# FFT filter and two MLPs: the transform's second transposition by transfers through device memory, the inverse with its table stationary, tables loaded once

## The chip, the cores and the metric

The kernel runs on 1 core of a Trainium2 chip. The metric is the time of one execution on the device in microseconds (us). In text and rows PE is TensorE, PEld its weight load, DVE is VectorE, ACT ScalarE, POOL GpSimd and SP SyncE. SP computes nothing here: it issues nearly all transfers, one after the other, in the order of its program.

## The reference

```python
def reference(x, filt_r, filt_i, ...):      # x (2, 3008, 256)
    X = np.fft.rfft(x, axis=1)
    Y = X * (filt_r + 1j * filt_i)[None]
    y = np.fft.irfft(Y, n=3008, axis=1).reshape(6016, 256)
    h = y @ moe_w_in                        # 256 -> 2048
    y = np.maximum(0.01 * h, h) @ moe_w_out # 2048 -> 256
    r = np.maximum(y @ moe2_w_in, 0.0)
    return (r * r) @ moe2_w_out
```

## The kernel before

The program is written out by hand, engine by engine. Each engine runs its own list in order, and semaphores are all that ties the lists together. An instruction that waits holds back everything behind it on its engine.

**The transform** works on 3008 = 64 x 47 points, in two halves of 128 channels, with both batches side by side.
- `over_n1(c, half)` (L763) multiplies four columns of X by a 128x128 DFT table `DM[:, 0]`; ACT (half 0) and DVE (half 1) copy the results to `TT1A`/`TT1B`. There are 12 chunks `c` per half (`CH`).
- Then come 32 units `i` (`UNITS`), 16 (`PAIRS`) for each half. A unit has, on PE, `turn` (L779, four transpositions), `spectrum` (L792, two matmuls with the forward table `TB` stationary) and `inverse` (L803, four matmuls with the data `YF` stationary and the inverse table moving). ACT copies `turn`'s result (`turned`, L444) and `inverse`'s (`back`, L448, into `UT`). DVE's `filtered` (L631) multiplies the spectrum by the filter in three instructions (L642, L646, L649), and POOL adds the two products (L373). PE's loop body `i` is `turn(i+3)`, `spectrum(i+2)`, `inverse(i)`.
- `turn_back(c)` (L815) transposes four 128x128 blocks of `UT`, ACT copies them to `V` (L455), `sequence(c)` (L824) multiplies them by the last DFT table, and DVE copies the result to `YT` (L652). There are 24 such chunks. Nine of half 0 stand in the middle, at `i == TURN` (16); a few stand in the last units; those up to c = 20 follow the loop; and the last three (`fill`, L968) stand between groups of the first MLP slot (`FILL` = 21).

**The weights of MLP 1** are prepared during the transform, for k = 0 to 7. SP loads `WIF` (L216), POOL forms sums in four instructions (`wi_sums`, L281: L287, L289, L292, L293), ACT rounds (`wi_round`, L459), and POOL forms the low part in three instructions (`wi_split`, L295: 384, 256 and 256 columns). The tables `WI_LOAD`, `WI_SUM`, `WI_HI` and `WI_LO` (L155 to L159) say after which unit each stands. For k = 0 to 5 the rounding stands at least two units ahead of the first split that needs it; k = 2 and 3 are done in the middle, beside the nine chunks.

**SP** keeps five filter slots. `load_filter(i)` (L204) waits for `inverse(i-5)` and loads the unit's table (`TB`, 182 KB) and its filter (`FL`, 224 KB). The tables come in twice, once for each half.

**The MLPs** are 96 slots of PE groups (L893 to L966). The first group needs POOL's linear forms of `YT` (`x_forms`, L328), ACT's roundings and DVE's differences (`x_split0`, L674).

Of the kernel before, what the change touches and what calls it, by code (L numbers as in the profile page):

```python
# [6 lines left out]
N1, N2 = 64, 47  # L7
# [17 lines left out]
FSLOTS = 5  # L25


def fft_mlp_kernel(nc, x, filt, dft, tab, w1i, w1o, w2i, w2o, out):
# [18 lines left out]
    YF = at("YF", [KR, 3, B, 2 * 128], f32, 24 * KB)  # L47
    XF = at("XF", [KR, 2, B, 2 * 128], f32, 30 * KB)
    UT0 = at("UT0", [128, B, MH, 128], f32, o_wo)
    V = at("V", [128, 2, 512], f32, o_wo + 24 * KB)  # L50
# [6 lines left out]
    UT1 = at("UT1", [128, B, MH, 128], f32, o_g)  # L57
    o_tb = [o_s + 2 * TBW * 4 * i for i in range(4)] + [o_x + 13824]
    TB = [at(f"TB{i}", [KR, 2, TBW], f32, o_tb[i]) for i in range(FSLOTS)]
# [24 lines left out]

    wi2 = nc.dram_tensor("wi2", [128, KU, 2, 7, 128], f32).ap()
    wo2 = nc.dram_tensor("wo2", [128, KU, 2, 2 * D], f32).ap()

    with ExitStack() as ctx:
        def sem(name):
# [8 lines left out]
        ft_in = [sem(f"ft_in{g}") for g in range(FSLOTS)]  # L98
        s2_ps = sem("s2_ps")
# [7 lines left out]
        v_ps = sem("v_ps")  # L107
        v_sb = sem("v_sb")
        y_ps = sem("y_ps")
        y_sb = sem("y_sb")  # L110
# [42 lines left out]
        TURN = PAIRS  # L153

        WI_LOAD = {0: 0, 2: 1, 6: 2, 9: 3, 12: 4, 14: 5, 20: 6, 23: 7}  # L155
        WI_SUM = {3: (0, 0), 4: (0, 1), 5: (1, 0), 6: (1, 1), 18: (4, 0), 19: (4, 1), 20: (5, 0), 21: (5, 1)}
        WI_HI = {5: 0, 7: 1, 20: 4, 22: 5}
        WI_LO = {7: (0, 0), 8: (0, 1), 9: (0, 2), 10: (1, 0), 11: (1, 1), 12: (1, 2),
                 22: (4, 0), 23: (4, 1), 24: (4, 2), 25: (5, 0), 26: (5, 1), 27: (5, 2)}  # L159
        FILL = 2 * CH - 3  # L160
# [4 lines left out]
        EARLY = CH - 3  # L165
        UT = [UT0, UT1]
# [30 lines left out]
        def _(sp):  # L197
# [6 lines left out]
            def load_filter(i):  # L204
                if i >= FSLOTS:
                    sp.wait_ge(u_ps, i - FSLOTS + 1)
                sp.dma_start(TB[i % FSLOTS][:, :, :], tab[:, i % PAIRS, :, :]).then_inc(ft_in[i % FSLOTS], 16)
                sp.dma_start(FL[:, i % FSLOTS, :, :], filt[:, i, :, :]).then_inc(ft_in[i % FSLOTS], 16)

            load_x(0)  # L210
            load_x(1)
            for i in range(UNITS):
                load_filter(i)
                if i - FSLOTS in WI_LOAD:
                    k = WI_LOAD[i - FSLOTS]
                    sp.dma_start(WIF[:, k, 0:4, :], w1i[:, k, :, :]).then_inc(wi_raw[k], 16)  # L216
# [57 lines left out]
        def _(pool):  # L274
# [53 lines left out]
            def x_forms(p, part):  # L328
# [4 lines left out]
                if part == 0:  # L333
                    if p == 0:
                        pool.wait_ge(y_sb, CH + 2)
                        pool.wait_ge(s2_ps, UNITS)
                    elif p == 1:
                        pool.wait_ge(y_sb, 2 * CH)
                    else:
                        pool.wait_ge(p3_ps, (p - 1) * KU)  # L340
# [29 lines left out]
            for i in range(UNITS):  # L370
# [3 lines left out]
                if i in WI_SUM:  # L374
                    wi_sums(*WI_SUM[i])
                if i in WI_LO:
                    wi_split(*WI_LO[i])
                if i == TURN:
                    for k in (2, 3):
                        for part in range(2):  # L380
                            wi_sums(k, part)
                    for k in (2, 3):
                        for part in range(3):
                            wi_split(k, part)
# [5 lines left out]
            for k in (6, 7):  # L390
                for part in range(2):
                    wi_sums(k, part)
            x_forms(0, 0)
# [3 lines left out]
            for k in range(2):  # L397
                wo_split(k)
                for part in range(3):
                    wi_split(6 + k, part)  # L400
# [27 lines left out]
        def y_bank(c):  # L428

            return c % 2 if c < FILL else 4 + c % 2  # L430
# [6 lines left out]
        def _(act):  # L437
# [10 lines left out]
            def back(i):  # L448

                j = 2 * (i % PAIRS)  # L450
                act.wait_ge(u_ps, i + 1)
                nc.scalar.activation(UT[i // PAIRS][:, :, :, 4 * j:4 * j + 8],
                                     PS[:, 4 + i % 2, 0:4 * K2].rearrange("p (b q m) -> p b m q", b=B, m=MH), ACT.Copy).then_inc(u_sb, 1)

            def turned_back(c):  # L455
                act.wait_ge(v_ps, c + 1)
                nc.scalar.activation(V[:, c % 2, :], PS[:, 6 + c % 2, :], ACT.Copy).then_inc(v_sb, 1)
# [22 lines left out]
            def x_round0(i):  # L480

                d, t = X0[i]
                if i == 0:
                    act.wait_ge(y_sb, CH + 2)
# [21 lines left out]
            for i in range(UNITS):  # L506
                if i + 3 < UNITS:
                    turned(i + 3)
                if i == TURN:
                    turned_back(0)  # L510
                if i == UNITS - 2:
                    turned_back(EARLY)
                    turned_back(EARLY + 1)
                if i == UNITS - 1:
                    turned_back(EARLY + 2)
                back(i)
                if i in WI_HI:
                    wi_round(WI_HI[i])
                if i == TURN:
                    for c in range(1, EARLY):  # L520
                        turned_back(c)
# [586 lines left out]
```

## Time and profile before

| | |
|---|---|
| median of 3 runs | 1106.75 us (1105.6 to 1107.02) |
| the profiled execution | 1106.98 us |
| its span | 1105.2 us |
| granted clock, mean | 1.000 |
| PE busy | 99% of the span |
| DVE, ACT, POOL busy | 70%, 52%, 27% |
| transform, to the first MLP group | 127.9 us |

The span runs from the first to the last instruction; the profiled execution's own time is 1.8 us longer. PE's busy share is near full in every stretch, so a wait on PE is a wait of the whole program. The other engines' shares are means over stages of different kinds. Times in the rows below are counted from the span's start.

### The profile page before, as it was taken

The numbers are of one execution on the slowest core, as the hardware profiler recorded it, in microseconds if no ns is written. First come the engines' busy times: TensorE is split into PE (matmuls) and PEld (weight loads), VectorE is DVE, ScalarE is ACT, GpSimd is POOL, SyncE is SP. The second block draws the span as 40 slices with busy tenths as digits, with TensorE's granted clock in tenths as the row PEclk, the third lists the DMA queues.
The fourth block names the chain that finished last, engine by engine and source line by source line (L and its number), as shares of the span: only waits on it lengthen the run. The fifth ranks groups of instructions, "written<-read, shape, count | busy, mean of one in ns | idle before, by whom it ended". The sixth has DMA issues, their size and how long they took to land.

```text
span 1105.2 us, 14486 instructions
## 1 busy us (share of the span) xinstructions
PE 1094.6 (99%) x5312; PEld 929.9 (84%) x5312; DVE 776.6 (70%) x1193; ACT 569.5 (52%) x991; POOL 301.3 (27%) x291
## 2 busy tenths in 40 slices
PE   8999999999999999999999999999999999999998
PEld 8899978888888888888888888888888888888887
DVE  2979787777677676776676667667666676677665
ACT  3455655565455555555554454554554554554543
POOL 0778833224334234234121120120120210210000
PEclk9999999999999999999999999999999999999999
DMA  8545110011211211212244200000000000000000
GB/s 311 165 150 171 45 43 1 1 50 46 48 51 51 60 44 41 65 39 51 58 157 148 81 1 1 39 1 1 39 1 1 36 1 1 39 1 1 39 1 36
DMA packets 64086, 58.34 MB, mean 53 GB/s; under 512 B 40592, under 2 KB 50960, under 8 KB 64016
## 3 DMA queue, kind: packets, MB, share of 16 engines
q1 hardware_dynamic: 63872, 57.23, 16.8%
q8 instruction: 42, 0.69, 0.3%
q14 instruction: 28, 0.23, 0.1%
q10 hardware_dynamic: 144, 0.20, 0.0%
HBM read 39.71 MB, written 17.69 MB: 52 GB/s over the span
## 4 chain that ended last, share of the span: by engine, by line
PE 98%; DVE 1%; DMA 0%; POOL 0%; issue 0%; ACT 0%; DVEq 0%
PE PS L879 16%; PE PS L880 16%; PE PS L881 16%; PE PS L887 13%; PE PS L889 13%; PE PS L888 13%; PE PS L799 2%; PE PS L811 2%; PE PS L770 2%; PE PS L832 2%; PE PS L788 1%; PE PS L821 1%; DMA DM<-in_dft 0%; POOL YF L373 0%; DVE GF L718 0%
## 5 line engine op out<-in xcount | busy, mean ns | idle before, releaser
L575 ACT ACTIVATE GH<-GF 128x512 fp32r<-128x512 f32 (+1 forms) x384 | 238.7, 622 | 224.8 <-DVE GF L720 116.3
L726 DVE TENSOR_TENSOR GL<-GF,GH 128x512 fp32r<-128x512 f32 (+1 forms) x384 | 259.6, 681 | 108.1 <-ACT GH L575 101.4
L880 PE MATMUL PS<-GL,WOH 128*128 128x512 f32 (+1 forms) x768 | 296.4, 386 | 0.0
L879 PE MATMUL PS<-GH,WOH 128*128 128x512 f32 (+1 forms) x768 | 296.3, 386 | 0.0
L881 PE MATMUL PS<-GH,WOL 128*128 128x512 f32 (+1 forms) x768 | 296.1, 386 | 0.0
L887 PE MATMUL PS<-XH,WIH 128*128 128x512 f32 (+1 forms) x672 | 260.1, 387 | 1.2 <-DVE GF L711 0.8
L889 PE MATMUL PS<-XH,WIL 128*128 128x512 f32 (+1 forms) x672 | 259.2, 386 | 0.0
L694 DVE TENSOR_TENSOR GF<-PS,GF 128x512 f32<-128x512 f32 (+1 forms) x96 | 65.3, 680 | 170.5 <-ACT GF L546 170.5
L881 PEld LDWEIGHTS PS<-GH,WOL 128*128 128x128 f32 x768 | 144.1, 188 | 27.7
L880 PEld LDWEIGHTS PS<-GL,WOH 128*128 128x128 f32 x768 | 144.1, 188 | 27.6
L879 PEld LDWEIGHTS PS<-GH,WOH 128*128 128x128 f32 x768 | 144.2, 188 | 27.6
L887 PEld LDWEIGHTS PS<-XH,WIH 128*128 128x128 f32 x672 | 126.1, 188 | 27.9 <-ACT SN L553 2.1
L888 PE MATMUL PS<-YL,WIH 128*128 128x512 f32 (+1 forms) x384 | 148.0, 385 | 0.0
L889 PEld LDWEIGHTS PS<-XH,WIL 128*128 128x128 f32 x672 | 126.1, 188 | 24.2
L546 ACT ACTIVATE GF<-PS 128x512 f32<-128x512 f32 (+1 forms) x96 | 56.6, 590 | 172.5 <-PE PS L881 172.5
L718 DVE SCALAR_TENSOR_TENSOR GF<-GF 128x512 f32<-128x512 f32 (+1 forms) x192 | 137.3, 754 | 1.7
L720 DVE SCALAR_TENSOR_TENSOR GF<-GF 128x512 f32<-128x512 f32 (+1 forms) x192 | 121.7, 674 | 1.7
L888 PE MATMUL PS<-XL,WIH 128*128 128x512 f32 (+1 forms) x288 | 111.1, 386 | 0.0
L360 POOL TENSOR_TENSOR YL<-YT,XH 128x1024 fp32r<-128x1024 f32 (+1 forms) x22 | 51.7, 2352 | 137.5 <-DVE GL L726 137.5
L569 ACT ACTIVATE GF<-PS 128x512 f32<-128x512 f32 (+1 forms) x96 | 56.7, 591 | 58.4 <-PE PS L889 58.4
L888 PEld LDWEIGHTS PS<-YL,WIH 128*128 128x128 f32 x384 | 72.1, 188 | 13.5
L344 POOL TENSOR_TENSOR XT<-YT 128x512 f32<-128x512 f32 (+1 forms) x12 | 15.2, 1268 | 188.3 <-DVE GL L726 185.2
(64 smaller groups left out, 1062.4 us busy)
## 6 DMA issues: line engine op xcount, KB each, us to landing
FL<-in_filt SPq DMA_DIRECT2D x32, 224.0 KB, 3.4
TB<-in_tab SPq DMA_DIRECT2D x32, 182.0 KB, 2.9
X<-in_x SPq DMA_DIRECT2D x8, 512.0 KB, 8.9
out_y<-YT SPq DMA_DIRECT2D x4, 1024.0 KB, 4.3
wi<-PWH SPq DMA_DIRECT2D x16, 224.0 KB, 2.5
wi<-PWL SPq DMA_DIRECT2D x16, 224.0 KB, 3.1
WIH<-wi SPq DMA_DIRECT2D x8, 448.0 KB, 3.4
WIL<-wi SPq DMA_DIRECT2D x8, 448.0 KB, 4.4
```

Of the source, the lines that this page charges most:

```text
L569: nc.scalar.activation(GF[:, g_slot(n), 0:width(s)], PS[:, XB[s % 2], 0:width(s)], ACT.Copy).then_inc(h_sb[UD], 1)
L575: nc.scalar.activation(GH[:, g, 0:width(s)], GF[:, g, 0:width(s)], ACT.Copy).then_inc(g_hi[kind], 1)
L694: nc.vector.tensor_tensor(h, PS[:, YB, 0:w], h, ALU.add).then_inc(h_sb[UA], 1)
L718: nc.vector.scalar_tensor_tensor(h, h, 0.01, h, ALU.mult, ALU.max).then_inc(g_sb[kind], 1)
L720: nc.vector.scalar_tensor_tensor(h, h, 0.0, h, ALU.max, ALU.mult).then_inc(g_sb[kind], 1)
L726: nc.vector.tensor_tensor(GL[:, g, 0:w], GF[:, g, 0:w], GH[:, g, 0:w].bitcast(f32), ALU.subtract).then_inc(g_lo[kind], 1)
L879: nc.tensor.matmul(acc, wh, xh, start=first, stop=False)
L880: nc.tensor.matmul(acc, wh, xl, start=False, stop=False)
L881: return nc.tensor.matmul(acc, wl, xh, start=False, stop=last)
L887: nc.tensor.matmul(acc, wh, xh, start=first, stop=False, skip_group_check=not first)
L888: nc.tensor.matmul(acc, wh, lo, start=False, stop=False, skip_group_check=not first)
L889: return nc.tensor.matmul(acc, wl, xh, start=False, stop=True, skip_group_check=not first)
```

## The change

- `inverse` has the inverse table stationary and `YF` moving: two matmuls of 256 columns in place of four of 96. Its result lies in PSUM with the point index on 96 partitions. ACT copies 96x512 (before 128x384) into `U`, a ring of four slots (`USLOTS`).
- `turn_back`, `UT` and ACT's `turned_back` are gone. SP stores each unit's `U` to device memory (`store_u`, 196 KB) and loads it back turned (`load_v`, six transfers of 512 KB for each half, in runs of 1 KB) into `V0` and `V1`. V0's loads stand beside units 18 to 28; V1's stand behind the loop, and the first of them waits for all stores of half 1.
- All 24 `sequence` chunks follow the loop (20 ahead of the MLP, `FILL` = 20, four in its first slot). They take two PSUM banks in turn; DVE copies the even chunks and ACT the odd ones.
- The 16 tables are loaded once (`TB`, 26.6 KB per partition, over the first batch of X). The first load waits for `over_n1`.
- The weights' preparation is spread evenly: `wi_sums(k)` at i = 5k+1 and 5k+2, `wi_round(k)` at 5k+3, `wi_split(k, 0)` at 5k+4, its other parts at 5k+5 and 5k+8, for k = 0 to 5. k = 6 and 7 follow the loop. Weight load k+1 stands at i = 5k+2; that of k = 7 stands behind the loads of V1.

```diff
@@ sync
             def load_filter(i):
+                if i < PAIRS:
+                    if i in (0, PAIRS - 2):
+                        for half in range(2):
+                            sp.wait_ge(n1_ps[half], CH // 2 if i == 0 else CH // 2 + 1)
+                    sp.dma_start(TB[:, i, :, :], tab[:, i, :, :]).then_inc(tb_in[i], 16)
                 if i >= FSLOTS:
                     sp.wait_ge(u_ps, i - FSLOTS + 1)
-                sp.dma_start(TB[i % FSLOTS][:, :, :], tab[:, i % PAIRS, :, :]).then_inc(ft_in[i % FSLOTS], 16)
                 sp.dma_start(FL[:, i % FSLOTS, :, :], filt[:, i, :, :]).then_inc(ft_in[i % FSLOTS], 16)
+            def load_w1i(k):
+                sp.dma_start(WIF[:, k, 0:4, :], w1i[:, k, :, :]).then_inc(wi_raw[k], 16)
+            def store_u(i):
+                half, u = i // PAIRS, i % PAIRS
+                sp.wait_ge(u_sb, i + 1)
+                sp.dma_start(zu[half, :, 2 * u:2 * u + 2, :], U[:, i % USLOTS, :, :]).then_inc(z_out[half][i % USLOTS], 16)
+            def load_v(half, g):
+                if g == 0:
+                    for u in range(USLOTS):
+                        sp.wait_ge(z_out[half][u], 16 * (PAIRS // USLOTS))
+                by_q = zu[half].rearrange("(m q) j e -> (q j) m e", q=4)
+                sp.dma_start(V[half][:, 4 * g:4 * g + 4, :, :].rearrange("p m b d -> p m (b d)"),
+                             by_q[:, 4 * g:4 * g + 4, :]).then_inc(v_in[half][g], 16)
...
+            for i in range(FSLOTS):
+                load_filter(i)
+            load_w1i(0)
             for i in range(UNITS):
-                load_filter(i)
...
+                if i + FSLOTS < UNITS:
+                    load_filter(i + FSLOTS)
+                store_u(i)
+                if i % 5 == 2 and i // 5 + 1 < KU:
+                    load_w1i(i // 5 + 1)
+                g = (i - PAIRS - 2) // 2
+                if i % 2 == 0 and 0 <= g < MH // 4:
+                    load_v(0, g)
+            for g in range(MH // 4):
+                load_v(1, g)
+            load_w1i(KU - 1)
+            sp.wait_ge(y_ps, CH)
             for k in range(KU):
-                sp.wait_ge(v_ps, CH)
-                if k >= 4:
-                    sp.wait_ge(y_ps, 2 * CH)
                 sp.dma_start(WOF[:, k, :], w1o[:, k, :]).then_inc(wo_raw[k], 16)
@@ scalar
             def back(i):
                 act.wait_ge(u_ps, i + 1)
...
+                if i >= USLOTS:
+                    n = i - USLOTS
+                    act.wait_ge(z_out[n // PAIRS][n % USLOTS], 16 * (n % PAIRS // USLOTS + 1))
+                nc.scalar.activation(U[:, i % USLOTS, :, :].rearrange("p k e -> p (k e)"), PS[0:K2, 4 + i % 2, :], ACT.Copy).then_inc(u_sb, 1)
...
+            for c in range(1, FILL, 2):
+                y_copy(c)
+                if c == 5:
+                    wi_round(6)
+                if c == 7:
+                    wi_round(7)
@@ tensor
             def inverse(i):
...
-                for b in range(B):
-                    for k in range(2):
-                        col = (2 * b + k) * K2
-                        mm = nc.tensor.matmul(PS[:, 4 + i % 2, col:col + K2], YF[:, i % 3, b, 128 * k:128 * k + 128],
-                                              TB[i % FSLOTS][:, k, KR:], start=True, stop=True)
+                for k in range(2):
+                    mm = nc.tensor.matmul(PS[0:K2, 4 + i % 2, 256 * k:256 * k + 256].rearrange("p (b d) -> p b d", b=B),
+                                          TB[:, i % PAIRS, k, KR:], YF[:, i % 3, :, 128 * k:128 * k + 128], start=True, stop=True)
...
+            def sequence(c):
+                half, g, b = c // CH, c % CH // 2, c % 2
+                pe.wait_ge(v_in[half][g], 16)
                 if c >= 2:
-                    pe.wait_ge(v_sb, c - 1)
+                    pe.wait_ge(y_sb[c % 2], c // 2)
...
+            pe.wait_ge(s2_sb, UNITS)
+            for c in range(FILL):
                 sequence(c)
```

Three places show how the order moves; the prediction speaks of each.

SP, from the last units to the weights of the second matrix, before (`TB`, `FL` tables and filter; `WIF`, `WOF` weights of MLP 1):

```order
L207 DMA TB_63<-in_tab 112x416
L208 DMA FL<-in_filt 112x512
L216 DMA WIF<-in_w1i 128x512
L207 DMA TB_64<-in_tab 112x416
L208 DMA FL<-in_filt 112x512
...
L222 DMA WOF<-in_w1o 128x512 x8
```

and of the change:

```order
L214 DMA zu<-U 96x512
L209 DMA WIF<-in_w1i 128x512
L214 DMA zu<-U 96x512
L221 DMA V_54<-zu 128x4x256
L214 DMA zu<-U 96x512 x3
L221 DMA V_55<-zu 128x4x256 x6
L209 DMA WIF<-in_w1i 128x512
L244 DMA WOF<-in_w1o 128x512 x8
```

The last `WIF` load (k = 7) stood ahead of the last three tables and filters, whose rows the ... leaves out in part; it now stands behind the last stores and the six loads of `V1`.

ACT, behind the loop, before (`V` copies of the transposed blocks, `WIH` the roundings of k = 6 and 7, `XH` of the MLP's input):

```order
L457 ACTIVATE V<-PS 128x512 x2
L461 ACTIVATE WIH<-WIF 128x896
L457 ACTIVATE V<-PS 128x512
L461 ACTIVATE WIH<-WIF 128x896
L457 ACTIVATE V<-PS 128x512
L487 ACTIVATE XH_73<-YT 128x512
```

and of the change (`YT` copies of the odd chunks):

```order
L483 ACTIVATE U<-PS 96x512 x3
L489 ACTIVATE YT<-PS 128x512 x3
L493 ACTIVATE WIH<-WIF 128x896
L489 ACTIVATE YT<-PS 128x512
L493 ACTIVATE WIH<-WIF 128x896
L489 ACTIVATE YT<-PS 128x512
```

ACT now frees a PSUM bank of `sequence` on both sides of the rounding of k = 7 (the second `WIH` row): the three copies and the single one ahead of it are those of c = 1, 3, 5 and 7, the one behind it is that of c = 9.

POOL in the loop, before (`YF` the addition of one unit, `WIL` splits), units 6 to 8:

```order
L373 TENSOR_TENSOR YF<-YF,XF 112x512
L292 TENSOR_TENSOR WIF<-WIF 128x128
L293 TENSOR_TENSOR WIF<-WIF 128x128
L373 TENSOR_TENSOR YF<-YF,XF 112x512
L299 TENSOR_TENSOR WIL<-WIF,WIH 128x384
L373 TENSOR_TENSOR YF<-YF,XF 112x512
```

and of the change, units 7 to 10:

```order
L314 TENSOR_TENSOR WIF<-WIF 128x128
L315 TENSOR_TENSOR WIF<-WIF 128x128
L396 TENSOR_TENSOR YF<-YF,XF 112x512
L321 TENSOR_TENSOR WIL<-WIF,WIH 128x256
L396 TENSOR_TENSOR YF<-YF,XF 112x512
L321 TENSOR_TENSOR WIL<-WIF,WIH 128x384
L396 TENSOR_TENSOR YF<-YF,XF 112x512
```

The 384-column split is the first part of a pair of weights, and waits for ACT's rounding of them. It now stands behind the addition of unit 9, one unit behind the one after which ACT rounds (8); it stood behind that of unit 7, two behind (5).

## Rows read from the trace of the kernel before

**Rows 1.** The page's busy line: us, share of the span, instructions.
```profile
PE 1094.6 (99%) x5312; PEld 929.9 (84%) x5312; DVE 776.6 (70%) x1193; ACT 569.5 (52%) x991; POOL 301.3 (27%) x291
```

**Rows 2.** Busy time by stretch, then granted clock, DMA share, GB/s.
```profile
45.47:56.00 10.53, 10.53 (x79) 9.54 (x79) 10.06 (x15) 6.72 (x12) 10.06 (x12) 1.00 0.71 216
```

**Rows 3.** Chain that ended last, 60 to 130 us: start, us, what.
```profile
70.08 0.44 PE PS L821 x4
70.52 0.89 PE PS L832 x8
...
83.03 0.87 PE PS L811 x8
...
107.01 0.87 PE PS L811 x8
...
114.01 0.92 PE PS L832 x8
...
127.24 0.91 PE PS L832 x8
```

**Rows 4.** Timeline of the last units: start, us, engine, line, instruction.
```profile
102.05 0.68 DVE L649 TENSOR_TENSOR XF<-PS,FL 48x512 f32<-48x512 f32 x1
102.81 1.28 POOL L373 TENSOR_TENSOR YF<-YF,XF 112x512 f32<-112x512 f32 x1 [0.31 <-DVE XF L649]
104.47 1.08 PEld L811 LDWEIGHTS PS<-TB,YF 112*128 112x128 f32 x8
104.68 1.03 PE L811 MATMUL PS<-TB,YF 112*128 112x96 f32 x8
105.75 0.49 ACT L452 ACTIVATE UT<-PS 128x384 f32<-128x384 f32 x1 [1.14 <-PE PS L811]
105.99 1.03 PE L799 MATMUL PS<-S,TB 96*112 96x256 f32 x4
106.19 0.59 ACT L446 ACTIVATE S<-PS 96x512 f32<-96x512 f32 x1
```

**Rows 5.** Timeline, weight preparation: a split in the loop, sums, a rounding.
```profile
99.58 1.00 POOL L299 TENSOR_TENSOR WIL<-WIF,WIH 128x384 fp32r<-128x384 f32 x1
...
112.71 0.45 POOL L287 TENSOR_TENSOR WIF<-WIF 128x128 f32<-128x128 f32 x1
...
114.19 0.46 POOL L293 TENSOR_TENSOR WIF<-WIF 128x128 f32<-128x128 f32 x1
...
117.18 0.94 ACT L461 ACTIVATE WIH<-WIF 128x896 fp32r<-128x896 f32 x1
```

**Rows 6.** DMA issues: queue, kind, count, KB each, median us to landing.
```profile
FL<-in_filt SPq DMA_DIRECT2D x32, 224.0 KB, 3.4
WIF<-in_w1i SPq DMA_DIRECT2D x8, 256.0 KB, 3.8
PVF<-in_w2o SPq DMA_DIRECT2D x16, 128.0 KB, 2.1
wo<-PVH SPq DMA_DIRECT2D x16, 128.0 KB, 1.7
```

**Rows 7.** DMA, 234 to 236 us: store of PVL, load of PVF, runs of 1 KB.
```profile
DMA packets 288, 0.26 MB, mean 131 GB/s; under 512 B 32, under 2 KB 288, under 8 KB 288
q1 hardware_dynamic: 288, 0.26, 39.6%
```

**Rows 8.** DMA, 15 to 27 us in 40 slices: X, then tables and filters.
```profile
GB/s 396 437 382 423 410 423 396 410 396 437 382 423 445 324 354 254 296 292 269 338 304 299 304 304 289 361 276 272 331 302 315 268 322 299 337 223 125 48 34 0
```

**Rows 9.** Timeline of the start: copies of the first N1 chunks.
```profile
6.79 0.60 ACT L442 ACTIVATE TT1A<-PS 128x512 f32<-128x512 f32 x1 [4.33 <-PE PS L770]
8.50 0.69 DVE L629 COPY TT1B<-PS 128x512 f32<-128x512 f32 x1 [8.50 <-PE PS L770]
10.21 0.60 ACT L442 ACTIVATE TT1A<-PS 128x512 f32<-128x512 f32 x1 [2.82 <-PE PS L770]
11.30 0.69 DVE L629 COPY TT1B<-PS 128x512 f32<-128x512 f32 x1 [2.11 <-PE PS L770]
```

**Rows 10.** Timeline: one sequence chunk, its DVE copy, POOL's first linear form.
```profile
117.81 1.06 PE L832 MATMUL PS<-DM,V 128*128 128x128 f32 x8
...
118.91 0.69 DVE L658 COPY YT<-PS 128x512 f32<-128x512 f32 x1 [0.64 <-PE PS L832]
...
119.68 1.28 POOL L344 TENSOR_TENSOR XT<-YT 128x512 f32<-128x512 f32 x1 [3.13 <-DVE YT L658]
```

**Rows 11.** Timeline: a wait of PE in the second MLP slot.
```profile
140.61 0.50 PE L887 MATMUL PS<-XH,WIH 128*128 128x512 f32 x1 [0.81 <-DVE GF L711]
```

More of the change, by code:

```diff
@@ L98, in fft_mlp_kernel @@
         ft_in = [sem(f"ft_in{g}") for g in range(FSLOTS)]
+        tb_in = [sem(f"tb_in{u}") for u in range(NJ // 2)]
         s2_ps = sem("s2_ps")
@@ L373, in _ @@
                 nc.gpsimd.tensor_tensor(YF[:, i % 3, :, :], YF[:, i % 3, :, :], XF[:, i % 2, :, :], ALU.add).then_inc(yf_sb, 1)
[L374 to L384, printed above, removed]
+                k, n = i // 5, i % 5
+                if n in (1, 2) and k < WI_EARLY:
+                    wi_sums(k, n - 1)
+                if n == 3 and k >= 1:
+                    wi_split(k - 1, 2)
+                if n == 4:
+                    wi_split(k, 0)
+                if n == 0 and k >= 1:
+                    wi_split(k - 1, 1)
+            wi_split(WI_EARLY - 1, 2)
             def beside_psum(s):
                 pool.wait_ge(g_lo[UB], s)
-            for k in (6, 7):
+            for k in range(WI_EARLY, KU):
                 for part in range(2):
                     wi_sums(k, part)
+            for k in range(WI_EARLY, KU):
+                for part in range(3):
+                    wi_split(k, part)
             x_forms(0, 0)
@@ L396, in _ @@
             x_split(0, 3)
-            for k in range(2):
-                wo_split(k)
-                for part in range(3):
-                    wi_split(6 + k, part)
+            wo_split(0)
+            wo_split(1)
             for k in range(2, KU):
@@ L508, in _ @@
                     turned(i + 3)
[L509 to L515, printed above, removed]
-                back(i)
[L517 to L521, printed above, removed]
-                        if c in (4, 5):
-                            wi_round(c - 2)
-            for c in range(CH, FILL + 1):
-                turned_back(c)
-                if c in (CH + 1, CH + 2):
-                    wi_round(c - CH + 5)
-                if CH + 3 <= c < CH + 6:
-                    x_round0(c - CH - 3)
-                if c == CH + 6:
+                back(i)
+                if i % 5 == 3 and i // 5 < WI_EARLY:
+                    wi_round(i // 5)
+            for c in range(1, FILL, 2):
[4 more added lines that the diff above has]
+                    wi_round(7)
+                if c == CH + 3:
+                    x_round0(0)
+                    x_round0(1)
+                if c == CH + 5:
+                    x_round0(2)
                     x_round(0, 2)
@@ L669, in _ @@
                     filtered(i + 2)
-                if i == TURN:
-                    for c in range(EARLY):
-                        sequence(c)
             def x_split0(i):
@@ L681, in x_split0 @@
                                         ALU.subtract).then_inc(x0_lo, 1)
-            for c in range(EARLY, FILL):
-                sequence(c)
-                if CH + 5 <= c < CH + 9:
-                    x_split0(c - CH - 5)
+            for c in range(0, FILL, 2):
+                y_copy(c)
+                if c == CH + 4:
+                    x_split0(0)
+            x_split0(1)
+            x_split0(2)
+            x_split0(3)
             def whole_a(s):
@@ L957, in down @@
                     pe.wait_ge(evac[t], p)
-                elif first:
-                    pe.wait_ge(y_sb, 2 * CH)
-                    pe.wait_ge(v_sb, 2 * CH)
+                elif first and t == 1:
+                    for y in y_sb:
+                        pe.wait_ge(y, CH)
                 pe.wait_ge(g_lo[kind], s + 1)
@@ L1044, in dft_tables @@
         inv[r, 0, inp], inv[IM + r, 0, inp] = w * c, -w * s
+    inv[:] = inv.reshape(KR, NJ, 2, 2, MH).transpose(0, 1, 4, 2, 3).reshape(KR, NJ, K2)
     return dft.astype(np.float32), tab.astype(np.float32), rows
```

141 lines of the change are left out of this document (47 added, 94 removed).

## The prediction

> **What bounds the kernel now.** I read the page's busy lines first: PE is busy for 99% of the span [rows 1], so a gain must take work from PE, and any wait that PE gets is paid in full. The change ends with the transform, so next I read the chain of waits there [rows 3]. It is PE nearly throughout. A unit of the loop takes 2.17 us. A chunk of the last stage takes 0.44 us for its four transpositions and 0.89 us for its matmuls. The last inverse ends at 114.0 us (I call this moment T), and the last chunk ahead of the MLPs ends at about 127.9. The timeline of a unit [rows 4] shows how near the others are. DVE's last product of unit 27 ends at 102.73, POOL adds until 104.09, and the inverse's weight load starts at 104.47, so POOL may come 0.38 us late. ACT copies the inverse's result at 105.75. The stretches [rows 2] show DVE and POOL at 96% in the loop and the DMA engines at 0.71 with 216 GB/s, so they are full near 305 GB/s.
>
> **The sum, part by part.** All times stand against the profiled execution (1106.98 us, 0.2 above the median).
>
> 1. The inverse with its table stationary streams 2 x 256 columns. It should take what `spectrum`, of the same form, takes: 1.03 us in the timeline, as the four of 96 columns do [rows 4]. It costs and gives nothing. ACT's copy becomes 0.59 for 0.49.
>
> 2. The transpositions go: 24 x 0.44 = 10.6 us of PE. By stages: the middle block (nine chunks of 1.33) goes from the loop, 12.0, and 0.4 more in the last units. Of what stands there most was filling, since the last additions wait for DVE, so no more than that is gained. T falls from 114.0 to 101.5. Then 20 chunks stand behind T.
>
> 3. The tables' first load waits until PE has six chunks of both halves behind it, near 17 us. X itself loads until about 20 us [rows 8], the table is small, and five pairs of table and filter (2.1 MB at 300 GB/s) are there by 27 us, when the first spectrum is due. Cost: nothing. If X were not the cover, the first units would wait.
>
> 4. POOL waits for ACT's rounding. Counted from the DVE end of unit 5k+3: its inverse starts at +1.74 and its copy at +3.02 [rows 4]. The copy takes 0.5 (it overlaps the next by 0.1) and the rounding 0.94 [rows 5], so it ends near +4.5. POOL has done its addition of unit 5k+4 at +3.5 and waits a us for this. Split (1.0) [rows 5], addition (1.28) and hand-overs end at +6.8, and the inverse of unit 5k+5 wants to start at +6.08. So PE waits 0.7 us, five times (k = 0 to 4) = 3.5. For k = 5 the split falls in the last units, where nothing is left ahead of PE: 1.0. Bounds: 0, if ACT's part hides somehow, and 0.9 each time. T = 106.0.
>
> 5. The weight load of k = 7 stands behind V1's six loads, its sums wait for it, ACT's `wi_round(7)` waits for the sums, and behind that stands ACT's copy of chunk 9, which frees the bank of chunk 11. So PE runs chunks 0 to 10 until about T+10.3 and stops. From T: copy 0.6; last store 2.0 (a 128 KB store lands in 1.7 [rows 6], 64 KB more are 0.2); V1's loads are issued at T+2.75. Six of 524 kB and the weights' 262 kB are 3.41 MB. The nearest rows, transfers in runs of 1 KB, moved 0.26 MB in 39.6% of 2 us, which is 330 GB/s [rows 7]: 10.3 us. What a load takes around its transfer is 2.1 less 0.4 = 1.7 [rows 6]. The weights land at T+14.8. Ends: 8.5 us at X's 400 GB/s, 11.4 at the tables' 300 [rows 8]. I take 330, since the run length is the same. Then four sums, 1.94 from the first's start to the last's end, rounding 0.94 [rows 5], copy 0.6: chunk 11 starts at T+18.3 and PE has stood for 8 us. This eats the gain nearly alone.
>
> 6. Chunks 11 to 19. PE needs 0.89 each, but two banks in turn bind it: matmuls 1.06, then DVE's copy 0.69 [rows 10], with hand-overs 1.8 to 1.95 for two chunks. I take 0.93: 8.4 us.
>
> 7. PE's clock after the stand. The only start from rest in the trace is the first: the copies of N1 chunks follow each other at 1.71 us (6.79, 8.50, 10.21), then at 1.09 [rows 9], and later chunks at 0.89. That is half pace, 1.2 GHz for 2.4, though the granted clock reads 1.00 for that stretch. Some 3.25 chunks at 1.71 for 0.93 cost 2.5 us. I take that; the other end is 0, if 8 us of rest do not do it. The Trainium skill (TensorE: Matmul & The Clock Gate, What's actually happening) says that the throttled state is the default, to which an idle PE returns and from which activity releases it. By that rule the stand inside the program costs the same 2.5 us as the start; without it, the sum would be 1111.5.
>
> 8. Behind chunk 14 the linear forms of the first MLP group (1.28 us each [rows 10]) have five chunks and one triple to hide in; the third form and the difference after it end about level with that. I put 0.5 for them. POOL is rid of the splits of k = 6 and 7 that stand beside DVE in the first slot, and with them PE's wait of 0.81 [rows 11]. Together -0.3. The four chunks in the first slot cost 3.6 as before (1.33 + 1.33 + 0.89).
>
> The first MLP group moves from 127.9 to 106.0 + 18.3 + 8.4 + 2.5 - 0.3 = 134.9, and nothing behind it changes: **+7.0 us, 1114.0 us**.
>
> **A rule against the change.** Its new loads read device memory in another order than it was written. The rows nearest to them, 1 KB runs at 330 GB/s [rows 7], show no penalty for short runs, and the loads keep runs of 1 KB. The Trainium skill (VectorE: DVE Perf Modes, The three transpose paths) calls a plain copy whose strides do the transposition 19 times slower than the transposing path when the inner stride is large, and recommends TensorE for 128x128. Its condition is not met here. Were it so all the same, V1 alone would take 19 x 10 = 190 us, near 1290; chance 0.01.
>
> **Rivals.**
> - *The transfers set the loop's pace.* A unit moves 186 (table) + 229 (filter) + 197 (store) + 52 (weights) = 664 kB in half 0, and 740 kB in units 18 to 28 with V0's 262 for the table. At 2.31 us a unit that is 287 and 320 GB/s, against 305 to 330 that the rows bear. Filters are asked for 6.2 us ahead and land in 3.4 [rows 6], so 2.8 us of lateness are free. If stores and loads together need 2.55 us a unit, 28 units are 6.7 late, less 2.8, and V1 comes 0.6 later: 1118.5. For it: the shares are near full. Against: V0's share lasts 12 units. Chance 0.15.
> - *POOL's waits cost nothing* (point 4): 1109.5. For it: ACT is idle most of the unit. Against: its place in the list is fixed. Chance 0.12.
> - *Faster: the last weights do not queue behind V1.* They are issued at T+5.4. If they land before T+6.9, nothing stops, there is no rest and no half pace, and the first group starts at 106.0 + 20 x 0.95 - 0.3 = 124.7: 1103.8. With the 3.8 us of a lone load [rows 6] they land at T+9.2, which gives 1105.9. It decides for "not slower" from a landing before T+10.3 (before T+8 if the clock falls). Against it: filters issued at 10 us landed only behind X. Chance 0.06.
> - *The inverse is no dearer or cheaper than read* belongs to point 1; were its two matmuls hindered by the weight loads, 0.1 a unit would add 3. Chance 0.02, near 1117.
>
> **How the numbers follow.** The main case has 0.64: 1109.7 to 1116 by the ends of points 4, 5 and 7. The time is 1114.0. The range 1108.5 to 1119.0 takes in the main case and the first two rivals and leaves out the faster one and the tails. What a measurement of this kernel can tell is 0.2%, 2.2 us. Faster: half of the third rival and its company with the second, 0.04. Same (1104.5 to 1109.0): the other half, and the lower part of the second rival, 0.10. Slower 0.86.
>
> **What would show it.** In the profile after: PE's inverse busy as before; a wait of ACT's rounding on POOL's sums of some 8 us or more, and one of PE on ACT's `YT` copy of about 8, at one place; the six V1 loads landing over about 10 us; chunk copies at 1.7 us spacing right after; waits of PE on POOL's addition of 0.7 us every fifth unit. I am wrong if PE's chunks run on without a stop, if the last weights land before T+10, or if the loop's units stretch by DVE waits on filters.

## The result, and the profile after

The change makes the kernel slower, by about twice what was predicted.

| us | before | after |
|---|---|---|
| median (runs) | 1106.70 (1105.6 to 1107.02, 4) | 1120.86 (1118.84 to 1122.46, 4) |
| ratio, 95% interval | | 1.0129 (1.0111 to 1.0147) |
| the profiled execution | 1106.98 | 1118.84 |
| its span | 1105.2 | 1116.8 |
| granted clock, mean | 1.000 | 0.994 |
| first inverse starts | 33.46 | 32.26 |
| T, end of the last inverse | 114.0 | 104.70 |
| first MLP group starts | 127.89 | 133.74 |
| from there to the span's end | 977.3 | 983.1 |

The forecast was 1114.0 (1108.5 to 1119.0). Profile against profile the loss is 11.9 us where 7.0 was forecast; the median of after lies 2.0 above its profiled execution, which the forecast did not foresee either. The last two rows of the table place the miss at once: the transform ends 5.85 us later (forecast 7.0), and another 5.8 us are lost behind it, where the forecast had nothing.

The two profiled executions do not start alike. The same first 168 matmul instructions, which the change does not touch, took 21.83 us in the one and 20.75 in the other:

```profile
4.68 21.83 PE PS L770 x168
4.55 20.75 PE PS L789 x168
```

Over all twelve profiles here they take 20.6 to 22.0 us, whatever the kernel, so over 1 us between two profiles can stem from the start alone. Counted from the first inverse, the first MLP group comes 7.05 us later than before (101.48 for 94.43), which is the forecast 7.0, and the loss by the profiles is 12.8. A part of the 2.0 between profile and median may be this quick start.

The busy line, which answers to [rows 1]: PE has 224 instructions fewer (96 transpositions, 128 of the inverse) and only 3.2 us less of busy time.

```profile
PE 1091.4 (98%) x5088; PEld 915.0 (82%) x5088; DVE 770.4 (69%) x1181; ACT 564.4 (51%) x979; POOL 298.1 (27%) x291
```

PE's waits: engine, tile and line, what it waited for, total us, times, longest.

```profile
PE PS L838 <- ACT YT L489: 6.7, 1, 6.7
...
PE PS L826 <- POOL YF L396: 4.5, 8, 1.8
PE PS L874 <- DVE YL L698: 2.4, 2, 1.4
PE PS L874 <- DVE GF L732: 1.4, 1, 1.4
PE PS L838 <- DVE YT L679: 1.1, 1, 1.1
PE PS L874 <- ACT GF L567: 0.4, 1, 0.4
```

Left out is the wait for the first load, 4.6 us as before. The first row is the stand that was predicted (point 5), the next the wait of every fifth unit and of the last units (point 4). The last four are in the first two MLP slots and were not predicted.

The chain of waits, by start, length and work, shows one wait in five units in full. L826 is the inverse, L321 the split, L396 the addition:

```profile
39.33 0.88 PE PS L826 x4
40.23 0.46 ACT U L483
40.73 0.95 ACT WIH L493
41.67 0.07 issue
41.74 1.00 POOL WIL L321
42.74 1.24 POOL YF L396
44.03 1.10 PE PS L826 x4
...
55.47 1.10 PE PS L826 x4
```

The inverse of unit 5k+3 is copied, ACT rounds, POOL splits and adds, and only then comes the inverse of 5k+5. Five units take 44.03 to 55.47, 11.44 us, where five times 2.17 are 10.85: 0.59 lost each time, by the path that point 4 names.

The chain behind the loop, from the last inverse to the chunks behind the stand:

```profile
103.13 1.55 PE PS L826 x4
104.70 0.60 ACT U L483
105.31 2.06 DMA zu<-U
107.45 0.38 SPq L221
...
111.61 7.98 DMA WIF<-in_w1i
119.66 0.46 POOL WIF L309
...
121.62 0.95 ACT WIH L493
122.57 0.49 ACT YT L489
123.07 0.14 issue
123.20 5.90 PE PS L838 x32
```

Copy, last store, V1's issues, the weights behind them, sums, rounding, copy of chunk 9, chunk 11: each link is there. The stores and V's loads, as in [rows 6], from the DMA issues (a filter's 224 KB now land in 3.9 us in the median, 3.4 before):

```profile
zu<-U SPq DMA_DIRECT2D x32, 192.0 KB, 3.5
V<-zu SPq DMA_DIRECT2D x12, 512.0 KB, 6.0
```

Granted clock by stretch (the seventh figure; before it the busy us of PE, PEld, DVE, ACT and POOL, behind it the DMA share and GB/s), where [rows 2] and all of before showed 1.00:

```profile
104.00:108.00 4.00, 4.00 (x23) 3.88 (x22) 0.69 (x1) 0.90 (x2) 1.49 (x4) 0.62 0.30 87
...
123.20:126.00 2.80, 2.80 (x13) 2.80 (x14) 0.00 (x0) 0.54 (x1) 2.80 (x5) 0.50 0.00 0
...
152.00:154.00 2.00, 2.00 (x6) 1.61 (x5) 1.70 (x4) 2.00 (x5) 0.00 (x0) 0.50 0.00 0
```

The clock fell three times: in the last units, where PE had just waited 1.79 and 0.80 us; behind the stand; and in the second slot. 0.50 is the level of 1.2 GHz. The longer of the waits in the last units:

```profile
101.23 1.10 PE L826 MATMUL PS<-YF,TB 112*96 112x256 f32 x4 [1.79 <-POOL YF L396]
```

The four chunks behind the stand took 5.90 us, 1.48 each.

The second slot and what leads to it, in the timeline (matmuls of the MLP L874 to L876 and L866 to L868, DVE's differences L698; idle time before and its releaser in brackets):

```profile
134.31 6.15 DVE L698 TENSOR_TENSOR YL<-YT,XH 128x512 fp32r<-128x512 f32 x3 [0.49 <-POOL XT L372]
...
136.04 0.50 PE L874 MATMUL PS<-XH,WIH 128*128 128x512 f32 x1 [1.35 <-DVE YL L698]
...
140.52 0.50 PE L874 MATMUL PS<-XH,WIH 128*128 128x512 f32 x1 [1.03 <-DVE YL L698]
...
142.54 1.08 PE L838 MATMUL PS<-DM,V 128*128 128x128 f32 x8 [1.06 <-DVE YT L679]
...
145.68 1.66 ACT L497 ACTIVATE WOH<-WOF 128x512 fp32r<-128x512 f32 x3
...
150.72 0.50 PE L874 MATMUL PS<-XH,WIH 128*128 128x512 f32 x1 [1.35 <-DVE GF L732]
...
152.42 0.63 PE L868 MATMUL PS<-GH,WOL 128*128 128x512 f32 x1
```

PE waits 5.2 us here in five places (1.35 + 1.03 + 1.06 + 0.38 + 1.35); in the kernel before its waits on the same engines, there, were 0.8 [rows 11] and 0.3. And where a matmul of 512 columns takes 0.40 us, those behind the last wait take 0.63: at half clock again, some 1.6 us over seven of them. Together this is the 5.8 us: 5.2 of waits less the 1.1 of before, and 1.6 of clock, make 5.7.

The four differences, as the minimum, median and maximum of their durations in ns, before (L680) and after (L698), and for one of each the POOL instruction beside it:

```profile
L680 DVE TENSOR_TENSOR YL<-YT,XH x4: 730/1164/2099, 124.7 to 130.4; 128x512 fp32r<-128x512 f32 x4
125.04 2.63 POOL L364 TENSOR_TENSOR XL<-XT,XH 128x1024 fp32r<-128x1024 f32 x1
126.12 2.10 DVE L680 TENSOR_TENSOR YL<-YT,XH 128x512 fp32r<-128x512 f32 x1
...
L698 DVE TENSOR_TENSOR YL<-YT,XH x4: 1331/1724/2855, 131.7 to 138.7; 128x512 fp32r<-128x512 f32 x4
135.58 2.64 POOL L387 TENSOR_TENSOR XL<-XT,XH 128x1024 fp32r<-128x1024 f32 x1
```

The difference beside the last row starts at 135.91 and ends at 138.77, 0.55 us behind POOL's end at 138.22; the one before ends at 128.22, 0.55 behind POOL's 127.67. It is so for all eight: each ends 0.54 to 0.56 us after the POOL instruction that ran when it started, however long that one was. DVE's copy from PSUM at 133.13, beside POOL's third form, took its usual 0.69.

### The profile page after: what moved, and what is told of

Read it like the earlier page. It is cut to its first block, busy times and chain, and to the rows that moved or that the text cites. A ratio compares the mean times of both kernels' runs of the same rounds, so it can differ in the third digit from the quotient of the medians.

```text
span 1116.8 us, 14070 instructions
## 1 busy us (share of the span) xinstructions
PE 1091.4 (98%) x5088; PEld 915.0 (82%) x5088; DVE 770.4 (69%) x1181; ACT 564.4 (51%) x979; POOL 298.1 (27%) x291
## 4 chain that ended last, share of the span: by engine, by line
PE 93%; POOL 2%; DMA 1%; ACT 1%; DVE 1%; issue 1%; SPq 0%; DVEq 0%
PE PS L867 15%; PE PS L866 15%; PE PS L868 15%; PE PS L874 13%; PE PS L876 13%; PE PS L875 13%; PE PS L789 2%; PE PS L826 2%; PE PS L816 2%; POOL YF L396 1%; PE PS L805 1%; DMA WIF<-in_w1i 1%; PE PS L838 1%; POOL WIL L321 1%; ACT WIH L493 1%
## 5 line engine op out<-in xcount | busy, mean ns | idle before, releaser
L866 PE MATMUL PS<-GH,WOH 128*128 128x512 f32 (+1 forms) x768 | 296.8, 386 | 0.0
L868 PE MATMUL PS<-GH,WOL 128*128 128x512 f32 (+1 forms) x768 | 296.6, 386 | 0.0
L874 PE MATMUL PS<-XH,WIH 128*128 128x512 f32 (+1 forms) x672 | 260.5, 388 | 4.1 <-DVE YL L698 2.4
L876 PE MATMUL PS<-XH,WIL 128*128 128x512 f32 (+1 forms) x672 | 259.3, 386 | 0.0
L868 PEld LDWEIGHTS PS<-GH,WOL 128*128 128x128 f32 x768 | 144.4, 188 | 27.8
L866 PEld LDWEIGHTS PS<-GH,WOH 128*128 128x128 f32 x768 | 144.3, 188 | 27.7
L874 PEld LDWEIGHTS PS<-XH,WIH 128*128 128x128 f32 x672 | 126.2, 188 | 31.2 <-DVE YL L698 3.3
L876 PEld LDWEIGHTS PS<-XH,WIL 128*128 128x128 f32 x672 | 126.3, 188 | 24.2
```

Source lines behind the costliest of these rows:

```text
L866: nc.tensor.matmul(acc, wh, xh, start=first, stop=False)
L868: return nc.tensor.matmul(acc, wl, xh, start=False, stop=last)
L874: nc.tensor.matmul(acc, wh, xh, start=first, stop=False, skip_group_check=not first)
L876: return nc.tensor.matmul(acc, wl, xh, start=False, stop=True, skip_group_check=not first)
```

## The experiments

All are the changed kernel with a part altered, unless said otherwise. They ran in three sets; the kernel before, run beside them, had medians of 1106.56, 1106.43 and 1106.28.

**1. The stand alone.** The load of the last weights, moved ahead of V1's:

```diff
+                if i == UNITS - 3:
+                    load_w1i(KU - 1)
...
-            load_w1i(KU - 1)
```

> Edit: the changed kernel with the load of the last pair of MLP weights (k = 7) issued beside unit 29, ahead of the loads of V1, and nothing else. Theory A (PE stands at chunk 11 because that load queues behind V1 and ACT's rounding of it stands ahead of a bank's copy): the stand of 6.7 us and the half-pace chunks behind it (2.3 us) go, so 1120.9 - 9 to 10 = 1111 us (1109 to 1113). Rival B (V1's own transfers are what the stage waits for, and the weights only happen to land last): PE now waits at chunk 12 for V1, gain under 3 us, 1118 or more.

Measured: 1112.63 (1112.3 to 1113.4), ratio 1.0052 (1.0040 to 1.0064). The chain:

```profile
104.43 1.71 PE PS L827 x4
106.14 15.64 PE PS L839 x120
```

15 chunks run without a stop, 1.04 each, and the stand is gone. It had cost 8.2 us by the medians (7.2 from T to the span's end in the two profiles, T being 106.1 here), more than the 6.7 that the wait itself shows.

**2. POOL's waits alone.** ACT's rounding one unit earlier:

```diff
-                if i % 5 == 3 and i // 5 < WI_EARLY:
+                if i % 5 == 2 and i // 5 < WI_EARLY:
```

> Edit: the changed kernel with ACT's rounding of weights k placed behind unit 5k+2 instead of 5k+3 (k = 0 to 5). Theory A (POOL's split of 384 columns waits for this rounding, and its additions come late for PE): the five waits of 0.6 us and about 1 us in the last units go: 1117 us (1116 to 1118.5). Rival C (POOL has too much work in the loop, 10.9 us in 10.85, whatever the order): its waits stay, gain under 1 us, 1120 or more.

Measured: 1118.52 (1117.34 to 1118.93), ratio 1.0102 (1.0088 to 1.0117), 2.3 less than the change, where 4 were expected. The five waits on POOL in the loop went as expected. What stays is nearly all of what PE waited in the last units (2.6 us in the changed kernel), so that the 1 us expected there did not come:

```profile
PE PS L826 <- POOL YF L396: 2.6, 5, 1.1
```

A part of the gain also went into the stand, since the last weights now landed at T + 15.7 and PE stood 7.6 us there.

DVE waits for a filter, 1.5 us at one unit near 91 us, where it was 0.6 in the profile of the changed kernel. That is not the faster loop's doing, or not alone. Experiment 1 has the loop of the changed kernel, and there too DVE waited:

```profile
DVE YF L666 <- DMA FL<-in_filt: 2.1, 3, 1.5
```

The transfers stand at a share of 0.98 and 314 GB/s in 80 to 100 us, and in the changed kernel at 0.99 and 320. So the rival that the transfers set the pace holds for one to three units late in the loop, in either form. Of this PE felt 0.5 us here and up to 0.7 at a time in the experiments that follow.

**3. Both, and the order of the chunks.** Experiments 1 and 2 together; in addition chunks 12 to 15 (the input of the linear forms) ahead of 8 to 11, with the roundings of k = 6 and 7, `x_round` and `x_split0`, and SP's wait ahead of the output weights, moved accordingly:

```diff
+        PERM = tuple(range(8)) + tuple(range(12, 16)) + tuple(range(8, 12)) + tuple(range(16, 2 * CH))
...
-                half, g, b = c // CH, c % CH // 2, c % 2
+                q = PERM[c]
+                half, g, b = q // CH, q % CH // 2, q % 2
...
-                if c == CH + 4:
-                    x_split0(0)
-            x_split0(1)
-            x_split0(2)
-            x_split0(3)
+                if c in (CH, CH + 2, CH + 4, CH + 6):
+                    x_split0((c - CH) // 2)
```

> Edit: both edits of the two runs before, the roundings of k = 6 and 7 behind chunks 1 and 3, and chunks 12 to 15 (first columns of half 1) computed ahead of 8 to 11, with all that waits for them moved by four chunks. Theory A (the 5.8 us lost in the first MLP slots come from the linear forms having only five chunks as cover): 10 + 4 + some 5 us less than the changed kernel, 1102 us (1100 to 1105), faster than the kernel before. Rival D (POOL and DVE slow each other there whatever the cover, so the chain of forms stays as long in the first slots): the last 5 us stay, 1107.

Measured: 1103.96 (1101.78 to 1106.9, 12 runs), ratio 0.9975 (0.9966 to 0.9984). The profiled execution took 1101.78 at a clock of 1.000. This beats the kernel before. PE's waits on the differences have gone, though the differences themselves still took 1.33, 1.67, 2.23 and 1.17 us beside POOL: what changed is what covers them. Behind T it still waits 1.4 us on DVE's `GF`, 0.8 on `YT` and 0.4 on ACT.

**4. Experiment 3 without the order,** that is 1 and 2 together, to price the order by itself.

> Edit: the changed kernel with the early load of k = 7 and the early roundings, chunks in their own order (so: the run with everything, without its order of chunks). Theory A (the linear forms of the first MLP group need more than the five chunks behind chunk 14 as cover, and PE then waits for DVE's differences): 4 to 6 us more than the run with everything, 1109 us (1108 to 1110.5), waits of PE on DVE's differences as in the changed kernel. Rival D (the last gain came from the two edits together, not from the order): within 1 us of it, 1104 us.

Measured: 1110.21 (1106.75 to 1111.26, 5 runs), ratio 1.0033 (1.0020 to 1.0046). The order, with the roundings that moved with it, is worth some 6 us of median. The spread is telling: the five executions took 1106.75 and 1107.53 at a mean clock of 1.000, 1110.21 at 0.997, and 1111.26 and 1111.14 at 0.995. The profiled one is the first. With no loss of clock its span is 4.1 us above that of experiment 3 (1104.1 for 1100.0). Of this 1.15 lie ahead of T, 0.8 of them ahead of the first inverse, where the two programs are the same. Behind T it is 2.95, and PE's waits there come to 5.3 us for 2.6, most of it by the differences:

```profile
PE PS L875 <- DVE YL L699: 2.4, 2, 1.4
```

So the order saves some 3 us of waits in the first slots, and the executions in which the clock fell as well took about 4 more.

**5 and 6. The clock alone.** The changed kernel with idle matmuls (they compute nothing that is used) ahead of chunk 11, so that PE does not rest: 28 of them, then 52.

```diff
+                if c == CH - 1:
+                    for k in range(52):
+                        nc.tensor.matmul(PS[:, 2, 0:128], V[0][:, 0, 0, :], DM[:, 1, :], start=True, stop=True)
```

> Edit: the changed kernel with 28 idle matmuls of 128 columns (their result is overwritten unread) ahead of chunk 11, where PE stands. Theory A (the half-pace chunks behind the stand are TensorE's clock after rest): chunks 11 to 14 keep the pace of 0.9 to 1.0 us instead of 1.5, the stand itself stays (the last weights land as before), 2.3 us less: 1118.6 us. Rival E (they are slow for another reason, such as transfers or POOL's work beside them): 1.5 us a chunk stay, 1120.9 us.

> Edit: the changed kernel with 52 idle matmuls ahead of chunk 11 (28 in the run before left PE at rest for 3.6 us after them). Their result is overwritten unread. They take 11.5 us, some 3 us more than the stand. Theory A (chunks 11 to 14 are slow because of TensorE's clock after rest): granted clock 1.00 behind the stand and 0.9 to 1.0 us a chunk. With chunk 11 starting about 3 us later and 2.3 us less behind it: 1121 to 1122 us. Rival E (another cause): four chunks still take 5.5 us, 1124 us.

Measured: 1120.7 (1120.04 to 1121.27), ratio 1.0124, and 1120.92 (1120.12 to 1122.39), ratio 1.0132. The first told nothing of itself: the weights landed at T + 17.2, PE still rested 3.6 us behind the 28, the granted clock was 0.78 in 124 to 128 and 0.80 in the four us after it, and the chunks took 5.50 us. With 52 the time is no better either, since they run on past the point at which chunk 11 could have begun; but the chain tells the two apart (L836 are the 52 idle matmuls, which the profile counts as two instructions each, L841 the chunks):

```profile
116.73 11.67 PE PS L836 x104
128.40 3.81 PE PS L841 x32
```

Four chunks take 3.81 us in place of 5.90, and their stretch shows the full granted clock:

```profile
128.00:132.00 4.00, 4.00 (x36) 3.87 (x35) 0.69 (x1) 1.14 (x2) 0.00 (x0) 1.00 0.37 102
```

So the slow chunks behind the stand are the clock, 2.1 us of it, and not bank hand-overs or the transfers; in the changed kernel the DMA share was 0.00 while the first of them ran (123.20 to 126.00).

**7. V0's loads out of the filters' way.** Experiment 3 with the last three of them at units 27 to 29.

```diff
-                g = (i - PAIRS - 2) // 2
-                if i % 2 == 0 and 0 <= g < MH // 4:
+                g = {PAIRS + 2: 0, PAIRS + 4: 1, PAIRS + 6: 2, UNITS - 5: 3, UNITS - 4: 4, UNITS - 3: 5}.get(i)
+                if g is not None:
                     load_v(0, g)
```

> Edit: the run with everything, and the last three loads of V0 issued beside units 27 to 29, behind the last filter, instead of units 24, 26 and 28. Theory F (late in the loop the transfers are full, and V0's loads push a filter 1.5 us past its time): DVE's wait for a filter goes, 1.5 us less, 1102.5 us. Rival G (the same bytes only move and V1 starts later by as much, or stores keep the queue full): the wait stays or comes back at chunk 12, 1104 us.

Measured: 1103.73 (1103.05 to 1107.93, 12 runs), ratio 0.9982 (0.9974 to 0.9990): no change, and DVE's wait for filters is still there, in the profiled execution larger:

```profile
DVE YF L668 <- DMA FL<-in_filt: 2.7, 2, 1.4
```

V0's loads are not its cause, or not alone; which transfer delays the filter stays open.

**8. The output weights' roundings.** Experiment 3, and ACT's `wo_round(0)` and `wo_round(1)`, which stood in one block with the third ahead of `g_round`, moved apart:

```diff
                     y_copy(FILL + 1)
+                    wo_round(0)
...
                     snap2(s)
+                if s == 0:
+                    wo_round(1)
...
                     y_copy(FILL + 3)
-                    wo_round(0)
-                    wo_round(1)
```

> Edit: the run with everything, and ACT's roundings of the first two output weights taken from behind the last chunk's copy to behind the copy of chunk 21 and behind the second snap, so that only one stands ahead of ACT's rounding of g in slot 1. Theory H (PE's wait of 1.35 us in slot 1 comes from the three roundings in a row, 1.66 us, ahead of that): the wait shrinks by about 1 us, 1103 us. Rival I (DVE's and POOL's work sets it, as in the kernel before, where PE waited 0.81 us at the same place): no change, 1104 us.

Measured: 1102.69 (1099.93 to 1105.63, 9 runs), ratio 0.9967 (0.9958 to 0.9976). The 1.4 us wait is gone; these are all of PE's waits but that for the first load and one of 0.2:

```profile
PE PS L827 <- POOL YF L398: 2.6, 5, 1.1
PE PS L840 <- DVE YT L683: 0.9, 1, 0.9
```

This is the best version that was found, 3.7 us faster than the kernel before.

**9. The same roundings without the order of the chunks** (experiment 4 and the edit of 8).

> The last weights ahead of V1, the roundings one unit earlier, and the two output-weight roundings apart (one behind the second fill copy, one behind snap2 of the first slot); the chunk order of the change is kept. It tells the wait for the output roundings from the one for DVE's differences. Theory S (the two are separate, one behind the other): the 1.4 us wait of PE on GF goes as it did in the version with the chunk order, the 2.4 us on DVE's differences stay, and the time is 1110.2 - 1.3 = 1108.9 (1107.5 to 1110). Theory T (one wait covers the other: ACT's roundings stand beside POOL's linear forms, and freeing the slot only lets PE run sooner into DVE's late differences): no change, 1110.2.

Measured: 1106.52 (1105.25 to 1109.54, 11 runs), ratio 1.0004 (0.9995 to 1.0012), below the range that theory S gave. The waits went as S says: those on `GF` are gone, the 2.4 us on the differences stay. But the median fell by 3.7, not 1.3. Most of these executions had a mean clock of 0.998, where three of five of experiment 4 had 0.995 to 0.997. The executions at a clock of 1.000 alone, 1105.64 here against 1106.75 and 1107.53, differ by 1.1 to 1.9, as S says. With the last wait of the second slot gone the clock seems to fall less, which fits and was not measured by itself.

**10. The control: the kernel before, with its output roundings moved apart likewise.**

> The kernel before, with the two output-weight roundings placed apart in the same way, nothing else. It tells what of the best version's gain belongs to the change. In the kernel before PE waited 0.81 us for GF in the second slot and 0.45 to 0.47 us at two places in the first. If these go: 1105.8 (1105.2 to 1106.4). If they stem from the fill chunks between the groups and not from the roundings: no change, 1106.5. Neither gives the 1102.7 of the best version with the transfers, so that the rest would belong to the change itself.

Measured: 1106.19 (1105.4 to 1107.92), ratio 1.0001 (0.9992 to 1.0010). No gain: the wait of [rows 11] went, but PE now waits for ACT, whose copies stand behind the roundings. The first of these waits was 0.3 before, the second is new:

```profile
PE PS L887 <- ACT SN L550: 0.7, 1, 0.7
PE PS L832 <- ACT V L457: 0.5, 1, 0.5
```

(The 0.45 and 0.47 us of the expectation were waits of PE's weight load. PE itself waited 0.28 us, once.) So the 3.7 us of experiment 8 are not to be had in the kernel before by this edit. No other order was tried there, but beyond the first load all of PE's waits in its profile come to 1.4 us (0.8, 0.3 and 0.3), and more than that no order can give by them.

The versions, in the order in which they were built up, against the 1120.86 of the change:

| kernel | median | step |
|---|---|---|
| the change | 1120.86 | |
| last weights ahead of V1 | 1112.63 | -8.2 |
| and roundings one unit earlier | 1110.21 | -2.4 |
| and output roundings apart | 1106.52 | -3.7 |
| and the chunks that the forms need first | 1102.69 | -3.8 |

They come from separate sets of runs, whose medians of before differ by 0.3 us.

## Why the prediction was wrong in size

Its direction and its path held; one term of the sum failed.

- **Point 1** (the inverse costs nothing): held. The loop's units take 2.17 us where nothing waits, the inverse 0.86 to 0.88 in the chain as [rows 3].
- **Points 2 and 4** (T = 106.0): T = 104.70, 1.3 early, and that is mostly the start of the execution. The first inverse began 1.20 us earlier than before, by chance. The wait of every fifth unit was 0.59 for 0.7, which makes 0.55, and the last inverse took 0.45 more at a fallen clock (1.55 for 1.10): -1.20 - 0.55 + 0.45 = -1.3. T is no firm number for the same two reasons. In the profiles of experiments 3, 4 and 8, with the same loop, it was 102.0, 103.2 and 104.2, but from the first inverse to T it was 69.96, 70.29 and 71.05, the last with 0.92 of fallen clock. The 1.0 of point 4 for k = 5 was not confirmed: with the rounding moved, PE's waits in the last units hardly changed (experiment 2), so point 2's 101.5 was about as much too low.
- **Point 3**: held. The first spectrum ran at 26.48 us, 1.20 earlier than before, and PE waited for no table; DVE waited for no filter until 92 us, and then 0.6.
- **Point 5**: held in its times. The weights landed at T + 14.9 (14.8 predicted), chunk 11 began at T + 18.5 (18.3). PE stood 6.7 us, not 8, since its chunks 0 to 10 took 12.06 us and not 10.3: the clock had fallen at 104 to 108. That changed nothing, because the chain ran through the transfers.
- **Points 6 and 7**: held in sum. Chunks 11 to 19 took 10.54 us (123.20 to 133.74), predicted 8.4 + 2.5 - 0.3. The clock's part is 2.1, by experiment 6.
- **Point 8 is the step that failed**, with the "nothing behind it changes" that follows it. It gave the forms "five chunks and one triple" to hide in, found the third form "about level", put 0.5 for them, took back 0.81 for the wait of [rows 11] and let nothing change behind. Measured, the program behind the first group lost 5.8 us. The runs show three things in its place:
  - *The cover did not suffice, and DVE was the engine.* The prediction gave POOL's forms a time and the differences (`x_split0`) behind them on DVE none. The four took 1.33, 1.68, 2.86 and 1.77 us, where in the kernel before they took 0.73, 2.10, 1.17 and 1.16; POOL works beside them both times, and each ends just behind POOL's instruction, not by its own length (see the rows of the first slot). The second waited for the third form until 134.31, when PE was already at its first group. This makes PE's waits of 2.4 us, and 1.1 more behind the same DVE. Experiments 3 against 4 and 8 against 9 make the order 3.8 to 6.3 us of median, and experiments 3 and 4 some 3 us where the clock did not fall.
  - *ACT's roundings of the output weights.* With all four fill chunks in the first slot the first two roundings fell behind the last copy and met the third: 1.66 us in one block ahead of `g_round`, and PE waited 0.38 and 1.35. Experiments 8 and 9: 1.3 to 3.7 us of median, 1.1 to 1.9 where the clock did not fall.
  - *The clock once more.* The same waits let it fall a third time, for some 1.6 us in the profiled execution. In experiment 4 the executions differ by this, about 4 us between those at a clock of 1.000 and the others. For the changed kernel itself that is not shown: its 1118.84 and 1122.46 have the same mean clock, 0.994.
- **The rivals.** POOL's waits did cost (0.59 each, not nothing). Last weights not queued behind V1: they were. The transfers set the pace: not in general, but late in the loop DVE waited for filters, 0.6 us in the profile of the changed kernel and 0.9 to 2.1 in those of experiments 1, 5 and 6 with the same loop. None of them was the cause of the miss. The stand was worth 8.2 us when the weights were moved ahead of V1; 6.7 of waiting and 2.1 of clock make 8.8, where points 5 and 7 had 8 and 2.5.

The rule of the Trainium skill that was weighed against the change (VectorE: DVE Perf Modes, The three transpose paths) had no effect here: the six loads of V1 and the weights, 3.41 MB, landed within 11.2 us (108.4 to 119.6), at 300 to 389 GB/s once under way. The other rule of the Trainium skill (TensorE: Matmul & The Clock Gate, What's actually happening) agrees with the trace: the granted clock of 0.50 behind 6.7 us of rest, and 1.00 with the rest filled.

What the prediction should have drawn on is a third. The Trainium skill (GPSIMD Engine Reference, Specifications) says that GpSimd's SBUF interfaces are shared with VectorE and contended by VectorE instructions with two SBUF inputs. `x_split0` is such an instruction. Its 0.73 to 2.86 us agree, and so does that each ends 0.54 to 0.56 us behind POOL's instruction. No run took POOL away from beside it.

What stays open: which transfer delays the filters near 91 us; how much of experiment 9's surplus is clock; and why the first 168 matmul instructions take 20.6 to 22.0 us.

## What to carry to other kernels

Where an edit moves work from one end of a serial chain of queues to the other, the stall inside it is easily found; look then at the consumers behind it, for each engine and not only the first (here POOL's forms, DVE's differences, ACT's roundings), and ask what covers each now. A load put in a queue behind megabytes that are needed later landed only with them, and moving that one load gave back 8.2 us. Time a DVE instruction that reads two tensors in SBUF while POOL works by the end of POOL's instruction, which set it in all twelve cases here, and not by its own size. And a wait of PE costs its length and can then cost the clock: take waits out to the last one before judging a change, since the same change was 1.3% slower as made and 0.33% faster once its queues were put in order.

## What the hardware showed beyond expectation

- Waits far shorter than the 6.7 us of the stand let the granted clock fall: 1.79 and 0.80 us in the last units were followed by 0.62 for 104 to 108 us, and several of 0.4 to 1.4 us in the first slots by 0.50 for 152 to 154. The same waits do not always do it. PE waited 1.07 to 1.08 and 1.03 to 1.04 us in the last units of experiments 3, 4, 8 and 9 alike; in the profiles of 3 and 4 the clock stayed at 1.00, in those of 8 and 9 it fell to 0.50 and the last inverse took 2.02 and 1.82 us for 1.10. Executions of one kernel differ likewise (1106.75 at 1.000, 1111.26 at 0.995).
- One and the same DVE operation with both inputs in SBUF took from 0.73 to 2.86 us, by what POOL did beside it: in the profiles of before, of the changed kernel and of experiment 3, twelve in all, it ended 0.54 to 0.56 us after the POOL instruction that ran when it started. With POOL mostly idle, DVE's `GL<-GF,GH` of the same size takes 0.68 in the mean.
- V's reads in runs of 1 KB reached 389 GB/s, above the 330 of [rows 7]:

```profile
GB/s 0 0 0 23 120 166 348 381 379 389 381 343 307 338 335 335 361 364 366 361 364 358 343 346 353 348 358 348 300 97 5 0 0 0 0 0 0 0 0 0
```

This is 107 to 123 us of the changed kernel in 40 slices.
